# Sixteen products on constants in front of one wait of PE, in the first batch's attention

## The reference

```python
scores = scale * np.matmul(q, k.transpose(0, 1, 3, 2))
cum = np.cumsum(np.log(np.clip(f, 0.0001, 1.0)), axis=-1)
decay = cum[:, :, :, None] - cum[:, :, None, :]
scores = np.where(causal, -1000000000.0, scores + decay)
attn = np.exp(scores - np.max(scores, axis=-1, keepdims=True))
attn = attn / (np.sum(attn, axis=-1, keepdims=True) + 1e-09)
x = np.matmul(attn, v)              # per head, then heads side by side
h = x @ w_in
x = (h * (1.0 / (1.0 + np.exp(-1.702 * h)))) @ w_out
# then, with phi, w1 and w2, the mixture of experts on x
```

## Time and profile before

| | us |
|---|---|
| median of 3 runs | 827.21 |
| lowest, highest | 824.52, 831.02 |
| the profiled execution | 831.28 |
| its span, first to last instruction | 829.5 |
| PE busy | 747.7 (90%) |
| DVE busy | 534.8 (64%) |
| ACT busy | 373.9 (45%) |
| POOL busy | 376.4 (45%) |

### The profile page before, as it was taken

The page is one execution under the profiler, slowest core; times in us unless marked ns, Lnnn a source line. Parts: engine busy times, 40 slices in busy tenths (PEclk is TensorE's granted clock), DMA queues, the critical chain, the costliest instruction groups (busy, mean ns, idle before and its releaser), DMA issues.

```text
span 829.5 us, 16692 instructions
## 1 busy us (share of the span) xinstructions
PE 747.7 (90%) x5865; PEld 695.6 (84%) x5865; DVE 534.8 (64%) x1430; ACT 373.9 (45%) x903; POOL 376.4 (45%) x394
## 2 busy tenths in 40 slices
PE   3788878999899898999999989999998999996996
PEld 2677778999899788998999889999998999993562
DVE  5888867777667767776777576867674434434323
ACT  4676754454545454545463454545443222111113
POOL 2344336465656255556474164747460766530000
PEclk9888879999999989999999699999997999998995
DMA  4333311333234213333334013333320455487986
GB/s 96 98 84 98 85 48 43 101 82 94 75 94 110 77 42 87 89 99 87 88 87 113 12 52 87 87 88 91 97 64 26 129 176 181 138 320 303 392 319 228
DMA packets 96517, 96.75 MB, mean 117 GB/s; under 512 B 61296, under 2 KB 61296, under 8 KB 96432
## 3 DMA queue, kind: packets, MB, share of 16 engines
q1 hardware_dynamic: 96432, 95.66, 38.4%
HBM read 90.84 MB, written 4.79 MB: 115 GB/s over the span
## 4 chain that ended last, share of the span: by engine, by line
PE 64%; DVE 15%; issue 7%; DMA 5%; ACT 4%; POOL 3%; SPq 1%; DVEq 0%; ACTq 0%; POOLq 0%
PE mb L1037 40%; PE xb L986 5%; PE yb L943 5%; PE zb L962 4%; PE mb L1012 2%; DVE prob L746 2%; DMA qk_in<-in_k 2%; DMA ring_b<-in_moe_w 2%; DVE qs L710 2%; DVE ptl L752 1%; DVE kl L714 1%; PE xb L923 1%; PE mb L1010 1%; PE yb L945 1%; PE zb L1132 1%
## 5 line engine op out<-in xcount | busy, mean ns | idle before, releaser
L1037 PE MATMUL mb<-xh,wih 128*128 128x288 f32 x512 | 161.6, 316 | 11.0 <-DVE hid L812 7.1
L1037 PE MATMUL mb<-gh,woh 128*128 128x288 f32 x512 | 158.1, 309 | 4.3 <-DVE hid L812 3.8
L1037 PE MATMUL mb<-xl,wih 128*128 128x288 f32 x512 | 153.4, 300 | 0.0
L1037 PE MATMUL mb<-xh,wil 128*128 128x288 f32 x512 | 153.2, 299 | 0.0
L1037 PE MATMUL mb<-gl,woh 128*128 128x288 f32 x512 | 151.4, 296 | 0.0
L1037 PE MATMUL mb<-gh,wol 128*128 128x288 f32 x512 | 151.3, 296 | 0.0
L570 POOL TENSOR_TENSOR wol<-stage,woh 128x512 fp32r<-128x512 f32 x64 | 82.5, 1289 | 122.8 <-DVE woh L704 122.8
L553 POOL TENSOR_TENSOR gl<-hid,gh 128x288 fp32r<-128x288 f32 x128 | 112.9, 889 | 53.6 <-ACT gh L635 52.3
L594 ACT ACTIVATE prob<-prob,m_row 64x576 f32<-64x576 f32 (+4 forms) x160 | 96.4, 604 | 61.3 <-DVE m_row L727 61.1
L570 POOL TENSOR_TENSOR wil<-stage,wih 128x512 fp32r<-128x512 f32 x64 | 82.6, 1290 | 88.0 <-DVE wih L704 88.0
L812 DVE SCALAR_TENSOR_TENSOR hid<-gate,mb 128x288 f32<-128x288 f32 x128 | 57.6, 452 | 98.1 <-ACT gate L641 96.6
(11 more groups left out here) (143 smaller groups left out, 1456.3 us busy)
## 6 DMA issues: line engine op xcount, KB each, us to landing
stage<-in_moe_w_in SPq DMA_DIRECT2D x64, 256.0 KB, 3.3
stage<-in_moe_w_out SPq DMA_DIRECT2D x64, 256.0 KB, 2.7
ring_a<-in_moe_w SPq DMA_DIRECT2D x16, 1024.0 KB, 7.6
ring_b<-in_moe_w SPq DMA_DIRECT2D x14, 1024.0 KB, 12.0
cum_b<-cum_dram SPq DMA_DIRECT2D x32, 288.0 KB, 4.2
qk_in<-in_q SPq DMA_DIRECT2D x32, 144.0 KB, 3.2
qk_in<-in_k SPq DMA_DIRECT2D x32, 144.0 KB, 3.8
v_in<-in_v SPq DMA_DIRECT2D x32, 128.0 KB, 3.2
```

What stands on the lines that cost most here:

```text
L1037: ins = mm(bank[:, 0:HALF], a[:, t, P * (j % 4):P * (j % 4) + P], x[:, t, cols], start=(i == 0), stop=(i == 11))
```

## The change

A step `fill` is put into PE's list, in the slots of the first batch from the second on, behind the last transpositions of probabilities and in front of `pv_first`. It is 16 products of `ident_r` (stationary, 128 x 128) with `mask_r` (moving, 128 columns) into bank 0 of mb. Nothing reads what they write. They wait for nothing and nothing waits for them, other than what stands behind them on PE.

```diff
--- before.py
+++ after.py
@@ -64,6 +64,7 @@
 INV_SQRT_D = DIM ** -0.5
 MASKED = 1e9
 GATE = 1.702
+FILL = 16
 EPS = 1e-9
 
 
@@ -144,7 +145,7 @@
             steps += [(0, ("split", slot - 3))] if 2 < slot < 7 else []
 
             if engine == "pe":
-                steps += pt(0) + pt(1) + score(1) + score(2) + qk + pt(2) + score(3) + pt(3) + pv_first + early + pv
+                steps += pt(0) + pt(1) + score(1) + score(2) + qk + pt(2) + score(3) + pt(3) + at(before, "fill", s - 1) + pv_first + early + pv
             elif engine == "act":
                 steps += (pt(0) + score(0) + pt(1) + score(1) + qk + pt(2) + score(2) + dup + pt(3) + score(3)
                           + norm + early_x + pv + xs[3])
@@ -963,6 +964,9 @@
                                  prob[:, par, POFF[i] + P * kt:POFF[i] + P * kt + P],
                                  swapped if back else ident)
                     ins.then_inc(p_tr, 1)
+                elif st[0] == "fill":
+                    for _ in range(FILL):
+                        mm(mb[:, 0, 0:P], ident_r[:, :], mask_r[:, :], start=True, stop=True)
                 elif st[0] in ("pv_first", "pv"):
                     s = st[1]
                     par = s % 2
```

## The result

The changed kernel takes 824.73 us (median of 20 runs, 816.68 to 828.57), the kernel before 830.85 us in as many (822.89 to 837.86). The ratio is 0.9947, with a 95% interval of 0.9925 to 0.9969: 0.53% faster, some 4.4 us. Ratios and their intervals compare fast executions alone, those within 1.5% of a kernel's fastest; the profiled ones of the first runs with 8, 32 and 4 fills were slow. The two medians themselves lie 6.1 us (0.74%) apart. The forecast was 821.3 us, 0.71% less than the median of three then known (827.21); its sign holds, and its size is near the upper end of the interval, 0.31 to 0.75%. In the profiled executions the span went from 829.5 to 821.7 us.

What follows compares the result with a forecast made beforehand. DVE was taken to set a floor near 9.4 us per first-batch head, with PE's falling clock lengthening slow stretches. Fill cost 0, clock gain 5.90 us and later effects 0 made 821.3 us from the 827.21 us median; range 816.5 to 828.5.

Steps and rivals of the forecast that it cites:

- what the clock gives back: Five slow stretches of the first batch return to full-clock length once PE's idle time is cut: 5.90 us gained together.
- The bound: First batch: DVE, busy 8.95 to 9.48 us per stretch, sets a floor near 9.4 us; PE's clock varies the rest.
- The fills' own time: Sixteen products before the first value product take 1.76 us, hidden by PE's wait for DVE's second split; cost 0 to 0.4 us.
- The model of 9.54 us: Full-clock length expected for the three slow first-batch stretches that hold a weight split on DVE: 41.41, 62.48 and 73.15.
- The model of 9.35 us: Full-clock length expected for the two slow first-batch stretches without a weight split on DVE: 83.72 and 94.02.
- The sum against the median: Whole kernel: the 5.9 us gain set against the three-run median of 827.21 us, giving 821.3 us.
- 1.57 us already left the clock full: PE's wait for DVE's second split: 1.57 us or less keeps full clock, 1.80 to 1.84 us is followed by 1.2 GHz.
- What PE did before the fall was to stand idle: At PE's wait for DVE's second split, the clock was full during the wait and half as fast when PE began again.
- A: First batch's slow stretches: PE is the bound and all slow time returns, 10.3 us, giving 816.9 us; chance 0.12.
- B: At the fills, narrow products count as too little work, so the clock falls anyway: 827.2 us; chance 0.13.
- C: Before each head's first value product, fills at low clock overrun the wait: 11.2 us lost, 838 us; chance 0.07.
- After the first batch: Low clock after the wait for the output's last split stays; counted as 0, at most 2.4 us either way.

## Which step of the prediction failed, and what held

*The step that failed* is the term "what the clock gives back", 5.90 us. It took the five falls of the clock in one execution for what the kernel loses in each. The mechanism behind it held, but the same five stretches gave back 4.96 us, and a second profile of the same kernel, hit in three stretches, lost so much less that the first batch as a whole gained 3.05 us against it and not 5.24. With the term fell its premise, that waits of 1.57 us keep the clock and those of 1.80 lose it, and the sentence that one per cent is about what a measurement can tell from no change: 20 runs of each kernel told 0.53% (0.31 to 0.75%).

*The bound.* Right: a loop of one head with DVE nearly full, and a PE clock that decides whether DVE waits. With the clock held, DVE's wait at the output's sum was gone in every head.

*The fills' own time.* Right: sixteen took 1.98 us with the last one's end, at full clock, and hid behind the wait; in two of eight heads the value products began 0.1 us later than usual (0.35 after line 715's end, not 0.25). The fills needn't be the reason: it happened in no head of the second profile of the change, and once in the second of the kernel before, which has none. The margin was thin all the same: with 32 the first batch ended 7.4 us later. With 16 no overrun showed.

*What the clock gives back, stretch by stretch.* 5.90 us were predicted, against the profiled execution. By the same stretches it was 1.72 + 0.96 + 0.90 + 0.58 + 0.80 = 4.96 us. The model of 9.54 us for a stretch with a weight split was the best case; with the clock full, the kernels here have 9.57 and 9.81 us in turn. The model of 9.35 us was wrong for the stretch from 83.72, which takes 9.8 us also at full clock. Small gains in front of and behind the five, and 0.13 us lost where the stretch had been at full clock, bring the first batch to 5.24 us; 0.28 of it lie in front of the first value product and aren't the fills' doing.

*The sum against the median.* I took the gain from one execution and subtracted it from the median of three. How often the clock falls differs from one execution to the next: five stretches in one profile of the kernel before, three in the other, whose first batch was 2.2 us shorter, though the two took 831.28 and 831.07 us in all. Against the second the change gains 110.64 - 107.59 = 3.05 us (3.3 with its own second profile). Two profiles can't say which is the more usual; the ratio of the 20 runs makes 4.4 us of it, their medians 6.1. The forecast time was 3.4 us too low for another reason: over 20 runs the median of the kernel before was 830.85 and not 827.21. That 830.85 - 5.90 = 824.95 comes so close to the measured 824.73 is luck, as the term was too large for the first batch.

*"1.57 us already left the clock full".* Here the reasoning was wrong though the forecast of a full clock was right. Eight waits of one profile seemed to split cleanly at 1.6 to 1.8 us. In the second profile waits of 1.80 and 1.81 left it full, and with four fills 1.4 us lost it in one profile and not in the other. The short waits may even be an effect: 1.57 us at 52.94 stands behind the slowest stretch (0.70), at whose end PE came late, and so do those of 1.54 and 1.57 in the kernel with less work on DVE and no fills, and the 1.30 of four fills (behind 0.71).

*"What PE did before the fall was to stand idle".* This was read in one stretch, from 94.02. In those from 41.41, 62.48 and 73.15 the clock was still full when PE began again, and fell only 0.2 to 1.2 us later (1.00 until 42.60, 0.50 from 42.65; a value product of 320 columns took 0.31 us at 42.38 and 0.47 at 63.21). The falls came during the waits or soon behind them.

*The chances.* Within 1%, to which I gave 0.76, is where it ended, but as a gain that is clear of noise and not as one that can't be told.

*The rivals.* A (all of the slow time back, 10.3 us) fell: half of the throttled time isn't what the stretch gets, since DVE's 9.3 us stand below it. So the rule from "TensorE: Matmul & The Clock Gate", Terms, in the Trainium skill overstates by a factor of two here (10.3 against 5.0 us in the five stretches). PE isn't alone on the path, and even PE's own busy time grew by less than the prediction said that the trace bears out: in the first three slow stretches it was 9.93, 8.41 and 8.40 us, where at full clock it is some 7.28, so 2.7, 1.1 and 1.1 us more; the rule gives 3.5, 1.7 and 1.8, probably because a part of the low clock fell on time in which PE waited. B (the clock falls all the same) fell by the profile after. C didn't happen with 16; with 32 its overrun did, at full clock.

*After the first batch.* The low clock behind the last wait was there again, 1.1 us longer (6.0 and not 4.9); it could be removed with 40 more fills. The remaining 2.5 us by which the profiled spans differ come from the later batches, where nothing was changed. Whether any of them is a consequence stays open: two profiles of the kernel before had 716.7 and 718.6 us from the mark to the end, two of the change 714.2 and 713.9, but other kernels with an unchanged rest reached from 711.3 to 725.5.

## What to carry to other kernels

Where a short wait of PE recurs in a loop, compare copies of the loop that ran at full and at half clock before costing anything: their difference is what a held clock is worth, and the next engine's busy time caps it. A fill must fit in the hole in front of the wait, at the full clock's spacing. By the end of the first batch, half of it gave the same here with more margin (its whole time didn't show it), a quarter did so in one profile of two, twice as much gave everything back, and the same products on the other side of the wait made the first batch 16 us longer than without any. And a gain read from one profile belongs to that execution: if the effect comes and goes between executions, take two profiles of the kernel before, or more.

## What the hardware did that I had not expected

The clock fell to 1.2 GHz around waits of only 1.8 us, once in a head of some ten us, and not around equal waits in the next heads of the same execution (1.81 us kept 1.00, 1.80 us gave 0.83). In one and the same program the number of heads hit was five of seven in one profile and three in another, which moved the first batch's end by 2.2 us. Four fills, which left waits of 1.4 us, had five heads hit in one profile and none in the other; eight and sixteen had none in two profiles each, nor in the three variants with sixteen.
